# One attention and two-MoE kernel: exponentials signalled singly, the block sums moved by a step, four weight loads moved back, soft weights read in longer runs

## The reference

```
scores_l = scale * np.matmul(q, k.transpose(0, 1, 3, 2))          # kept where |i - j| < 16
scores_s = scale * np.einsum('bhsd,bhnd->bhsn', q, k_sum) + log(32)
a = softmax(concatenate([scores_l, scores_s]));  x = a @ concatenate([v, v_sum])
```

## Time and profile before

| | |
|---|---|
| median of three runs | 380.62 us |
| profiled execution | 383.07 us |
| its span | 381.3 us |
| PE busy | 326.8 us (86%) |
| DVE busy | 175.7 us (46%) |
| ACT busy | 143.3 us (38%) |
| POOL busy | 100.5 us (26%) |
| bytes moved by DMA | 81.64 MB |

### The profile page before, as it was taken

The page is one execution under the profiler, slowest core; times in us unless marked ns, Lnnn a source line. Parts: engine busy times, 40 slices in busy tenths (PEclk is TensorE's granted clock), DMA queues, the critical chain, the costliest instruction groups (busy, mean ns, idle before and its releaser), DMA issues.

```text
span 381.3 us, 9001 instructions
## 1 busy us (share of the span) xinstructions
PE 326.8 (86%) x3268; PEld 233.1 (61%) x3269; DVE 175.7 (46%) x406; ACT 143.3 (38%) x329; POOL 100.5 (26%) x181
## 2 busy tenths in 40 slices
PE   1879879889898979969967798799999999999991
PEld 0566656666676743232316156588888888888880
DVE  2677867877875551370105686332322323223231
ACT  1576666766766331311000081232331323313221
POOL 5666575676764000000000000211212212122121
PEclk9999999999999998998986999899999999999998
DMA  8999999999999625999940820101011011010110
GB/s 308 355 422 409 416 421 417 420 419 421 398 392 408 261 77 193 348 391 404 394 178 10 337 98 0 57 28 55 37 46 55 28 55 46 37 55 28 55 55 33
DMA packets 23851, 81.64 MB, mean 214 GB/s; under 512 B 2312, under 2 KB 2312, under 8 KB 21776
## 3 DMA queue, kind: packets, MB, share of 16 engines
q1 hardware_dynamic: 20928, 74.13, 49.7%
q0 software_dynamic: 1920, 6.29, 4.3%
q10 hardware_dynamic: 976, 0.87, 0.7%
HBM read 74.99 MB, written 6.29 MB: 213 GB/s over the span
## 4 chain that ended last, share of the span: by engine, by line
PE 56%; DMA 16%; DVE 12%; POOL 4%; ACT 4%; issue 4%; SPq 3%; ACTq 0%; DVEq 0%; POOLq 0%
PE ps L900 32%; DMA ring<-in_vt 11%; DMA ring<-in_moe_w 5%; PE ps L630 3%; PE ps L886 3%; POOL ring L503 3%; PE ps L643 3%; PE ps L600 3%; SPq L285 2%; ACT work L958 2%; PE ps L785 2%; PE ps L744 2%; PE ps L698 2%; DVE ps L1119 2%; PE ps L651 1%
## 5 line engine op out<-in xcount | busy, mean ns | idle before, releaser
L900 PE MATMUL ps<-high_w2b,hid_high 128*128 (+1 forms) x184 | 72.5, 394 | 4.1 <-DVE hid_low L1363 4.1
L900 PE MATMUL ps<-low_w2b,hid_high 128*128 (+1 forms) x184 | 72.5, 394 | 0.0
L900 PE MATMUL ps<-high_w2b,hid_low 128*128 (+1 forms) x184 | 72.2, 392 | 0.0
L958 ACT ACTIVATE work<-ps,small 128x120 f32<-128x120 f32 x192 | 53.7, 367 | 39.8 <-DVE small L1123 39.5
L556 POOL DMA_INDIRECT out_x<-work,small x24 | 23.5, 979 | 150.0 <-DVE small L1356 60.3
L1363 DVE SCALAR_TENSOR_TENSOR hid_low<-ps,hid_high 128x1024 fp32r<-128x1024 f32 x26 | 31.8, 1225 | 57.5 <-ACT hid_high L1053 57.5
L1035 ACT ACTIVATE work<-ps,small 128x512 f32<-128x512 f32 x24 | 16.5, 689 | 98.0 <-PE ps L900 98.0
L900 PEld LDWEIGHTS ps<-high_w2b,hid_high 128*128 128x128 f32 x184 | 35.0, 190 | 11.6 <-issue 4.6
L600 PE MATMUL ps<-ident,work 128*120 128x128 f32 x192 | 31.8, 289 | 10.8 <-ACT work L958 10.5
L900 PEld LDWEIGHTS ps<-high_w2b,hid_low 128*128 128x128 f32 x184 | 35.0, 190 | 7.5
L900 PEld LDWEIGHTS ps<-low_w2b,hid_high 128*128 128x128 f32 x184 | 34.9, 190 | 6.7
(11 more groups left out here) (228 smaller groups left out, 369.5 us busy)
## 6 DMA issues: line engine op xcount, KB each, us to landing
ring<-in_moe_w SPq DMA_DIRECT2D x13, 2048.0 KB, 12.9
ring<-in_qk SPq DMA_DIRECT2D x16, 1104.0 KB, 14.6
ring<-in_v SPq DMA_DIRECT2D x16, 780.0 KB, 10.2
ring<-in_moe_w SPq DMA_DIRECT2D x12, 512.0 KB, 11.3
ring<-in_vt SPq DMA_DIRECT2D x7, 384.0 KB, 9.2
comb<-in_vt SPq DMA_DIRECT2D x7, 384.0 KB, 8.1
x_or_g<-in_moe_w SPq DMA_DIRECT2D x1, 2048.0 KB, 8.9
whole_w2b<-in_moe_w SPq DMA_DIRECT2D x4, 512.0 KB, 8.5
```

What stands on the lines that cost most here:

```text
L900: last = pe.matmul(ps[:, 4 + u, :], hidden_part[:, u, m * P:(m + 1) * P], matrix[:, bass.ds(e * UNIT + m * DM, DM)], start=m == 0 and i == ...
L958: last = act.activation(probs[u][:, j, :], sc[u][:, j // 2, (j % 2) * KC:(j % 2 + 1) * KC], ACT.Exp, bias=negmax[u][:, j:j + 1], scale=flo ...
```

## The change

Five edits in one.

- **Exponentials.** Each of the four exponentials raises `exp_done` by one, and each transpose of `probs_T` waits for its own. Before, the last one raised it once for all four.
- **Block sums.** The PE transpose L608 and the DVE copy L1136 move from step 0 of the pair to step 1, and POOL does halve(n+1) ahead of fill_sums(n).
- **Early units.** Units 0 to 3 are all issued behind the last loads of q, k, vT and v.
- **Weight layout.** A partition takes four neighbouring rows of a matrix in place of every 128th, so that a w1 unit is read in runs of 16 KB (before 4 KB), a w2 unit in runs of 8 KB (before 2 KB), the last two units in runs of 4 KB (before 2 KB). For this, PE reads every fourth column of `si_sb` (L716) and of `h_sb` (L773) as its weights.
- **One wait.** L716 waits for both halves of `si_sb` at its start.

```diff
-    EARLY_BEHIND = ((1, 1), (2, 1), (3, 3), (3, 3))
+    EARLY_BEHIND = ((3, 3),) * 4
...
-            eng.dma_start(unit_of(kidx).rearrange("p (c n) -> p c n", n=t.shape[2]),
-                          t[e].rearrange("(c p) n -> p c n", p=P)).then_inc(unit_loaded[kidx], 16)
+            halves = 1 if t is w1 else 2
+            eng.dma_start(unit_of(kidx).rearrange("p (f r) -> p f r", f=halves),
+                          t[e].rearrange("(f p c) n -> p f (c n)", f=halves, p=P)).then_inc(unit_loaded[kidx], 16)
+
+        def every_fourth(rows, c):
+
+            return rows.rearrange("p (q c) -> p c q", c=DC)[:, c, :]
...
-                              t[e].rearrange("(f m p) n -> p f m n", f=2, p=P)[:, f, 2 * half:2 * half + 2, :])\
+                              t[e].rearrange("(f p m) n -> p f m n", f=2, p=P)[:, f, 2 * half:2 * half + 2, :])\
...
+            fill_sums(0)
             halve(1)
-            fill_sums(0)
             for n in range(1, B * NPAIR):
                 fill_gaps(n)
-                fill_sums(n)
                 if n + 1 < B * NPAIR:
                     halve(n + 1)
+                fill_sums(n)
...
-                pe.wait_ge(exp_done, b * NSTEP + s + 1)
                 for j in range(4):
+                    pe.wait_ge(exp_done, (b * NSTEP + s) * 4 + j + 1)
                     last = pe.transpose(pt[s % 2][0:KC, j, :], probs[s % 2][:, j, :], ident[:, :])
...
-                if g == 0:
+                if g == 1:
                     ahead_pair(sums_by_block, b, pair + 1, u)
...
-                if c % 2 == 0:
-                    pe.wait_ge(si_ready, c // 2 + 1)
-                last = pe.matmul(ps[:, 1, c * SLOTS:(c + 1) * SLOTS], si_sb[:, c * P:(c + 1) * P], selr,
+                if c == 0:
+                    pe.wait_ge(si_ready, 2)
+                last = pe.matmul(ps[:, 1, c * SLOTS:(c + 1) * SLOTS], every_fourth(si_sb, c), selr,
...
-                    last = pe.transpose(ps[:, 2 + pr % 2, m * P:(m + 1) * P], h_sb[pr % 2][:, m * P:(m + 1) * P],
+                    last = pe.transpose(ps[:, 2 + pr % 2, m * P:(m + 1) * P], every_fourth(h_sb[pr % 2], m),
...
-                    last = act.activation(probs[u][:, j, :], sc[u][:, j // 2, (j % 2) * KC:(j % 2 + 1) * KC], ACT.Exp,
-                                          bias=negmax[u][:, j:j + 1], scale=float(D) ** -0.5)
-                last.then_inc(exp_done, 1)
+                    act.activation(probs[u][:, j, :], sc[u][:, j // 2, (j % 2) * KC:(j % 2 + 1) * KC], ACT.Exp,
+                                   bias=negmax[u][:, j:j + 1], scale=float(D) ** -0.5).then_inc(exp_done, 1)
...
                 dve.wait_ge(av_done, b * NSTEP + s + 1)
-                if g == 0:
+                if g == 1:
                     ahead_pair(copy_block_sums, b, pair + 1, u)
```

## The result

The changed kernel takes 386.44 us (median of 4 runs, 385.83 to 387.76) against 380.3 us of the kernel before beside it: ratio 1.0143, interval 1.0107 to 1.018. So it is 1.4% slower. The forecast was 383.9 us, 0.9% slower, with its own range up to 386.7.

What follows compares the result with a forecast made beforehand. Attention was taken as bound by a ring of waits through VectorE, ScalarE and TensorE, the soft MoE by DMA. Attention +6.1, layout -2.1, weight reads 0, clock -0.7 gave +3.3: 383.9 us, own range 382 to 386.7, 8-in-10 377.0 to 387.3.

Steps and rivals of the forecast that it cites:

- The ring: Attention: waits through VectorE, ScalarE and TensorE set the pair's pace; moved copy and transpose lengthen it from 6.63 to 7.29 us.
- The last batch: Attention's last batch, without loop registers: pairs go from 6.43 to 6.89 us, +0.9 us over 2 rounds.
- The start: Pair 1 of attention: values wait for fill_sums until about 24.3 us, step 1 at 26.5 against 25.00, +1.5 us.
- The stalls: Attention: TensorE's two later waits at L608 for GpSimd's halving, 2.64 us, taken as gone; other bound, they stay.
- Attention as a whole: End of attention: start, longer rounds, removed stalls and about 1.0 us back from the last pair give +6.1 us.
- Early units: Seven weight units loaded before the logits, in by some 140 us, needed beyond 155: no cost; without that cover 10 us.
- The layout: Soft MoE weight loads: longer runs cut seven units from 37.4 to 35.1 us; taken as -2.1 us, bounds 0 and -4.
- Rival D: Soft MoE loads: longer runs do not speed DMA, all else as forecast, 386.0 to 386.7 us; counted within the forecast's 0.58.
- Weights read apart: TensorE's strided weight loads at L716 and L773: taken as 0; if twice as long, at most 3.7 us.
- rival C: Strided weight loads at L716 and L773 take twice as long, +3.7 us, all else as forecast: 387.6 us; chance 0.12.
- The clock: Last L785: without TensorE's stall the lower granted clock may not follow; taken as -0.7 us, bounds 0 and -1.4.
- The sum: Whole kernel: +6.1 - 2.1 + 0 - 0.7 = +3.3 us, 386.4 us profiled, 383.9 us on the median, 0.9% slower.

Runs made afterwards that it cites:

- e2: Kernel before with only the block sums moved to step 1 and GpSimd's new order (halve ahead of fill_sums): 387.45 us, ratio 1.0150.
- e5: Changed kernel with the block sums' transpose and copy back in step 0, GpSimd's new order kept: 379.92 us, ratio 0.9957 to the kernel before.
- e6: Changed kernel with the sums' transpose L613 still in step 1 but ahead of the wait for pT_ready: 384.06 us, ratio 1.0074 to the kernel before.
- e11: Kernel before with single exponentials, late early units and weight layout, plus an unread 32 x 128 VectorE copy heading step 1: 380.33 us, ratio 0.9998.
- a2: Second measurement of the changed kernel without any edit: 387.52 us against 381.25 us of the kernel before, ratio 1.0181.
- e3: Kernel before with only units 0 to 3 issued behind all loads of q, k, v: 379.17 us, ratio 0.9924.
- e9: Kernel before with single exponentials, late early units, weight layout, and ScalarE writing si_sb and h_sb sorted: 376.58 us, ratio 0.9885.

## Why the prediction was right, and where its sizes were off

**The ring.** Right in its mechanism. The copy and L613 entered the ring in step 1 and take their time there: e2 has the loss alone, e5 removes it, e6 and e11 give each piece its share. The term was +0.66 us in a round and measured +0.52. Of the three segments the first (1.40 + 0.42) and the last (2.64 - 0.09 + 0.33) came out within 0.02 us: 1.82, and 2.54 + 0.34. The middle one was taken over as 2.59 and is 2.30. The prediction had read it as VectorE without a gap. These are VectorE's rows in the kernel before that follow the maximum at 88.82, and the rows of the same pair, the tenth, in the changed kernel:

```profile
89.53 0.16 DVE L1123 TENSOR_SCALAR small<-ps 128x4 f32<-128x4 f32 x1
89.75 0.95 DVE L1114 TENSOR_REDUCE small<-ring 128x24 f32<-128x768 f32 x1
90.74 0.18 DVE L1150 RECIPROCAL small<-ps 128x4 f32<-128x4 f32 x1
...
93.75 0.66 DVE L1123 TENSOR_REDUCE ps<-ps 128x4 f32<-128x480 f32 x1
94.67 0.95 DVE L1118 TENSOR_REDUCE small<-ring 128x24 f32<-128x768 f32 x1
95.53 0.17 DVE L1154 RECIPROCAL small<-ps 128x4 f32<-128x4 f32 x1
96.20 0.66 DVE L1123 TENSOR_REDUCE ps<-ps 128x4 f32<-128x480 f32 x1
```

The block maxima begin 0.93 us behind the maximum, after the change 0.92 us; `attended` begins 0.99 us behind them, after the change 0.86 us. The second gap held a wait: L630 began at 90.00, and `attended` began 0.74 us behind it, as it does at 87.42 and 88.16 in step 1. After the change L635 of step 2 begins at 93.76, 1.77 us before `attended`, and the wait is gone. Two paths of nearly equal length met there, and the copy used up part of the difference: of the 2.59 us 2.45 are left. In the ninth pair the same wait was longer. There the block maxima begin early in both kernels (0.78 and 0.77 us behind the maximum), `attended` began 1.16 us behind them (84.11) and now begins 0.87 us behind them, and 2.61 us became 2.30. So the wait of 0.1 to 0.3 us hid that much of the copy's cost, and that is why pairs of one length became pairs of 7.00 and 7.14 us. e11 shows the same in the tenth pair (2.45 instead of 2.52). Why the block maxima begin sooner in some pairs than in others isn't known.

**The last batch.** +0.54 us over two rounds instead of +0.92: periods of 6.70 us for 6.89. The last pair gave back 0.9 us, as forecast 1.0.

**The start.** The values of step 0 waited for `fill_sums` until 24.50, forecast 24.3. Step 1 was forecast at 26.5. It came at 27.43; the granted clock was at its lower level of 1.2 GHz (0.50) from 26.1 to 29.5 us, behind the 2.43 us in which TensorE stood, and L635 of step 1 took 1.14 us instead of 0.69. In a2 (2.41 us) and in e6 a stretch of the same length begins at 24.6 and at 24.1. In e2, where TensorE stood 1.80 us, there is none, and step 1 came at 26.45. So the new wait seems to have a second price, which the prediction had not counted: 0.9 us here, 1.6 us in a2 (28.10). That the wait brings the stretch is read from these four traces and not tested by itself.

**The stalls.** Right: no wait of L613 for GpSimd is left in the changed kernel. (In pair 0 one of 1.22 us, at 15.52, has become one of 1.33 us of the scores for `fill_gaps`, at 16.29.) The price of 2.64 us stands in e3's trace as 2.0 us at the end of attention and in its runs as 2.9 us.

**Attention as a whole**: +5.1 us for +6.1. The rounds with their stalls gone brought +3.0 for +4.6, the start +2.4 for +1.5.

**Early units.** Right: they cost nothing. Between 126 and 205 us the changed kernel's list of waits has none for a DMA, and that of the kernel before has only the one of the earlier trace rows.

**The layout.** -2.1 us and the clock's -0.7 make -2.8; measured, from the first L778 to the end of the last w2 matmuls, 202.83 - 164.90 = 37.93 us against 41.17, so -3.2. The wait of 2.09 us is gone, and the last w2 matmuls are all at the full clock, 3.64 us for 32. The 423 GB/s of the sum stood in no row; measured were 416 and 425. Rival D falls: longer runs do speed DMA here (416 and 425 GB/s, 408 and 381). The time alone would not have told so: D had put it at 386.0 to 386.7, and 386.44 lies in there.

**Weights read apart.** Taken as 0, bounded by 3.7 us; here rival C was partly true. The eight loads of L721 take 329 ns instead of 192 and its matmuls 2.08 us instead of 1.08: +1.0 us on the path, since VectorE, and L749 behind it, wait for them. The sixteen of L778 take 211 ns instead of 140, which makes a group of four 0.75 us instead of 0.66, +0.3 us together. The term was read from the wrong end. At L721 a load is 137 ns longer and the matmuls come 125 ns further apart, so nearly nothing of it is hidden beside them; at L778 it is 71 ns longer and four matmuls take 90 ns more. That this is so because a matmul of L721 has 32 columns and one of L778 128 is likely and wasn't tested. The Trainium skill says that each access which crosses to a new line of 16 bytes pays ("SBUF — State Buffer", the note on cachelines), and the trace agrees: loads with that step take 1.7 and 1.5 times as long.

**The clock.** -0.7 us was taken for a stretch that vanishes. It did, and others came: 26.1 (3.4 us long), 155.8 (3.4) and 241.2 (6.8) where before had 142.8 (3.4), 197.5 (3.4) and 241.8 (3.4). Three more are in both traces, a few us apart: 170.2 and 176.3 (3.4), 204.3 and 207.0 (6.8), and one that lasts to the end. Together they are 24 us before and 28 us after. L749 beside 155.8 took 8.34 us for 7.07, while L703, which had 7.05 us before, took 5.36. The forecast could say that the stretch behind one stall goes, and not where others come. The runs of one kernel show what this is worth. The version e9 took 374.0 us at a mean granted clock of 0.977 and 379.1 us at 0.960. So 2.8 us between two profiled executions and 6.1 us between the medians are no contradiction: the profiled execution of before took 383.07 us where its timed runs took 379.97 to 381.54.

**The sum.** On the profiled execution the forecast was +3.3 us and the traces show +2.8. The terms that were off have both signs and nearly cancel: the rounds -2.0 (loop -1.6, last batch -0.4), the last pair +0.1, the start +0.9, the weight loads of L721 +1.0, the layout -0.4 (in which those of L778 lie), and the wandering clock (L703 -1.7, L749 +1.3, and +0.4 behind L809, with 3.4 us more at the lower level from 241.2 on). That the sum came within 0.5 us is therefore partly luck. That the median came 2.5 us above the point forecast is the other matter: the sum was made against an execution 2.8 us above its median and carried over to the median unchanged. That the clock alone made this difference is likely by its size and not shown.

## What to carry to other kernels

An engine that is busy 46% of the time can set the pace: follow one period from row to row through all the engines until the parts add up to it, and only then ask whether a moved instruction lands inside or outside. An operation of 0.3 us that is free in one step cost 0.7% (trace) to 1.0% (runs) in the next, and a program with a lead of its own work (here L613) should place it in front of the wait that ends last, not behind. A segment that is read as "no gap" should be checked for a wait at the start of each of its rows. If a layout makes a DMA's runs longer, let the engine that writes the intermediate do the sorting, not TensorE's weight load: here ScalarE's reads of PSUM with a step of four values cost nothing by its rows (688 ns), though the gain of 1.3 us is too small for the runs to tell.

## What the runs showed of the hardware

- Loads of 128 x 128 float32 weights with a step of 16 bytes took 329 ns instead of 192 (L721) and 211 ns instead of 140 (L778).
- ScalarE read PSUM with the same step at no cost: 688 ns for 128 x 512 float32 with and without it.
- A stall of 2.43 us on TensorE at the start was followed 1.6 us later by 3.4 us at the lower granted clock, one of 2.41 us (a2) 0.2 us later; one of 1.80 us in the same place (e2) was not.
- Weights in runs of 16 and 8 KB came at 408 to 438 GB/s in pieces of 4 us, in runs of 4 and 2 KB at 385 to 413.
- The same program (e9), run again, took 374.0 and 379.1 us, with a mean granted clock of 0.977 and 0.960.
